# One more chunk of w_out's remainders on VectorE, two ScalarE steps moved to later units, and the order main, rest in the last sums and stores

## The chip, the cores and the metric

The kernel runs on one core of one Trainium2 chip. The metric is the device time of one execution in microseconds (us); 1128.37 us is the median of three runs of the kernel before. Durations below come from one profiled execution of it.

## The reference, cut to what matters

```python
w = softmax(weight_gen, axis=-1)                # (4, 4096, 8 heads, 7 taps)
x_unf[b, s, k] = x_pad[b, s + k]                # 7 causal taps over the sequence, zeros ahead of it
x = einsum('bshk,bskhg->bshg', w, x_unf)        # dynamic convolution, 24 channels a head
x = x.reshape(16384, 192)
h = x @ w_in                                    # (192, 2048)
g = h * (1.0 / (1.0 + exp(-1.702 * h)))
out = g @ w_out                                 # (2048, 192)
```

All inputs and outputs are float32.

## The kernel before, in words

The 16384 tokens are cut into 18 pieces: four narrow ones (512 tokens) and fourteen wide ones (1024 tokens). The hidden dimension is worked off in units. A unit is a 128-row chunk of the hidden dimension for 1024 columns; a narrow piece has 8 units and holds two chunks side by side in each, a wide one has 16. Unit n counts over the whole program, 0 to 255; v counts within a piece.

Matmuls take float32r operands, so each float32 operand is split in a rounded part (hi) and a remainder (lo = value - hi), and a product is hi*hi + hi*lo + lo*hi. For w_in (w1 in the code) and w_out (w2) this split is made in the kernel, in the first units, while the products already run. w2 has 16 chunks, held as two groups q of eight; the narrow pieces' unit n uses chunk n of both groups. A chunk of w2 is 192 columns: 128 for the main accumulator, 64 for the rest accumulator. "One chunk" in an index range like `w2_of(first, last, ...)` always means that chunk in both groups.

TensorE, per unit: `first_product(n)` (L633, the matmuls of L663, 18 pairs into hid) and, two units later, `second_product(n - 2)` (L667, matmuls of L679, 20 into acc_main and acc_rest). Its order at the start is first products 0, 1, 2, second 0, first 3, second 1, first 4, second 2, first 5, second 3, first 6, second 4, first 7, second 5, 6, 7, first 8. `second_product(n)` waits for unit n's `gate_lo`, and in its first units for the remainders of w2 (L683 to L686).

ScalarE, per unit: gate (L318) and gate_hi (L321) from hid, in order; behind them in certain units come extra steps. Unit 0: it rounds w2's chunks 4 to 7. Units 2 and 4: it copies two quarters of w1's late remainders into w1_lo (L333). Unit NEG_AT = 2: it writes the negated rounded chunks SOON to 7 of w2 (L337). Unit ADDED_AT = 5: it waits for the two transfers below and rounds their result into w2's remainder columns (L343), main and rest. VectorE, per unit: gate_lo (L577), then shares of the convolution of the pieces to come, in the order of a written list (STEPS_AT, STREAM); in unit 2 also `w2_remainder(2, 4)` (L470).

GpSimd only issues transfers there. After the negation (w2_negated) it issues two accumulating transfers (L608), one for each q, that add the negated rounded chunks to the raw ones and so leave raw - rounded; a similar one for w1's late half is issued at 14.3 us (L605). SyncE issues, in order: w1_hi doubled across the halves (L211, L212), w1_lo doubled (L215, L216) once `w1_late_ready` is 2, the taps of all later pieces (L200) once w2_lo_ready and w2_late_ready are complete, because they overwrite the raw weights, and then the windows of x (L248) and the output stores.

The last piece's last three units (REST_FIRST = 13) sum rest crosswise, main straight, rest straight, main crosswise. The end is then: ScalarE copies acc_rest's upper half (L358), VectorE adds the lower one (L561), ScalarE copies both main halves (L362), and stores go out as rest 0, main 0, rest 1 on SyncE (L236 to L243) and main 1 on ScalarE's queue (L364). All other units use main straight, rest crosswise, main crosswise, rest straight.

Of the kernel before, what the change touches and what calls it, by code (L numbers as in the profile page):

```python
# [5 lines left out]
P = 128  # L6
# [3 lines left out]
ACT = mybir.ActivationFunctionType  # L10
AX_X = mybir.AxisListType.X

HALF = 64
LANES = 32
NARROW, WIDE = 8, 16
PIECES = 4 * (NARROW,) + 14 * (WIDE,)
N = WIDE * LANES
# [1 line left out]
LAG = 2  # L19
SLOTS = 4  # L20
EVICT_AT = 1
REST_FIRST = 13
NEG_AT, ADDED_AT = 2, 5
MAX_AT, EXP_AT = 2, 3

STEPS_AT = ((0, 3, 5, 2, 4, 2, 2, 2),
# [12 lines left out]
def ffn_of_dynamic_conv(nc: bass.Bass, x_runs: bass.AP, tap_runs: bass.AP, x_first: bass.AP, tap_first: bass.AP,  # L39
# [15 lines left out]
    CH, D = w2_rows.shape[1:]  # L55
# [11 lines left out]
    LAST = len(PIECES) - 1  # L67
    START = [sum(PIECES[:j]) for j in range(len(PIECES) + 1)]
# [5 lines left out]
    with ExitStack() as ctx:  # L74
# [76 lines left out]
        def wait(eng, s, value):  # L151
            if value > 0:
                eng.wait_ge(s, value)
# [18 lines left out]

            return (k + h) % SLICES

        SOON = CH // 4
        LATE = slice(FH // 2, FH)
        MAIN, MAIN_LO = slice(0, P), slice(2 * P, 3 * P)
        REST_COLS, REST_HI, REST_LO = slice(P, 2 * P), slice(P, D), slice(D, 2 * P)
# [3 lines left out]

        def turned(j):
            return prod[:, 1, 0:PIECES[j] * CB].rearrange("p (k n) -> p k n", k=SLICES)

        def last_cols(h):
            return slice(2 * LANES * START[LAST] + h * N, 2 * LANES * START[LAST] + (h + 1) * N)

        def own(j, part):

# [6 lines left out]
        @block.sync  # L197
        def _(sp):
            def load_taps(first, last, s):
                sp.dma_start(taps[:, tap_span(first, last)], tap_runs[:, tap_span(first, last)]).then_inc(s, 16)  # L200

            sp.dma_start(taps[:, tap_span(0, 0)], tap_first).then_inc(taps_loaded[0], 16)
            sp.dma_start(x_head, x_first).then_inc(x_loaded, 16)
            sp.dma_start(w1_raw, w1_rows).then_inc(w1_loaded, 16)
            sp.dma_start(w2_raw, w2_rows).then_inc(w2_loaded, 16)
            sp.dma_start(ident[:], identity).then_inc(ident_loaded, 16)
            load_taps(1, 3, taps_loaded[1])
            sp.dma_start(xwin[:, 0:NARROW + HALO, :], x_runs[:, START[1]:START[2] + HALO, :]).then_inc(x_added, 16)

            sp.wait_ge(w1_hi_ready, 1)  # L210
            sp.dma_start(w1_hi[LOWER, :, 1, :].bitcast(F32), w1_hi[UPPER, :, 0, :].bitcast(F32)).then_inc(w1_doubled, 16)  # L211
            sp.dma_start(w1_hi[UPPER, :, 1, :].bitcast(F32), w1_hi[LOWER, :, 0, :].bitcast(F32)).then_inc(w1_doubled, 16)  # L212
            sp.wait_ge(w1_lo_ready, 3)
            sp.wait_ge(w1_late_ready, 2)
            sp.dma_start(w1_lo[LOWER, :, 1, :].bitcast(F32), w1_lo[UPPER, :, 0, :].bitcast(F32)).then_inc(w1_doubled, 16)  # L215
            sp.dma_start(w1_lo[UPPER, :, 1, :].bitcast(F32), w1_lo[LOWER, :, 0, :].bitcast(F32)).then_inc(w1_doubled, 16)  # L216
            sp.wait_ge(w2_lo_ready, 4)
            sp.wait_ge(w2_late_ready, 2)
            load_taps(4, LAST, taps_loaded[2])

            def store(j):
                cols = slice(2 * LANES * START[j], 2 * LANES * START[j + 1])
                if is_narrow(j):
                    sp.wait_ge(main_summed, j + 1)
                    sp.wait_ge(main_out_dve, j + 1)
                    sp.dma_start(out[0:P, cols], outs_main[:, 0, :]).then_inc(main_stored, 16)
                    sp.wait_ge(rest_summed, 2 * (j + 1))
                    sp.dma_start(out[P:D, cols], outs_rest[:, 0, :]).then_inc(rest_stored, 16)
                else:
                    sp.wait_ge(main_out_act, j + 1)  # L230
                    sp.wait_ge(main_out_dve, j + 1)
                    sp.dma_start(out[0:P, cols], outs_main[:].rearrange("p h n -> p (h n)")).then_inc(main_stored, 16)
                    sp.wait_ge(rest_out, 2 * (j + 1))
                    sp.dma_start(out[P:D, cols], outs_rest[:].rearrange("p h n -> p (h n)")).then_inc(rest_stored, 16)

            def store_last():  # L236

                sp.wait_ge(rest_out, 2 * LAST + 1)
                sp.dma_start(out[P:D, last_cols(0)], outs_rest[:, 0, :]).then_inc(rest_stored, 16)
                sp.wait_ge(main_out_act, LAST + 1)  # L240
                sp.dma_start(out[0:P, last_cols(0)], outs_main[:, 0, :]).then_inc(main_stored, 16)
                sp.wait_ge(rest_out, 2 * LAST + 2)
                sp.dma_start(out[P:D, last_cols(1)], outs_rest[:, 1, :]).then_inc(rest_stored, 16)  # L243

            def load_window(j):

                sp.wait_ge(conv_ready, j - 1)
                sp.dma_start(xwin[:], x_runs[:, START[j]:START[j] + WIN, :]).then_inc(x_reloaded, 16)  # L248

            load_window(2)  # L250
            for j in range(LAST):
                if j + 2 <= LAST and j >= 2:
                    load_window(j + 2)
                store(j)
            store_last()
            sp.wait_ge(main_stored, 16 * (LAST + 2))
            sp.wait_ge(rest_stored, 16 * (LAST + 2))

        @block.scalar
        def _(act):  # L260
# [50 lines left out]
            for j in range(LAST + 1):  # L311
                for v in range(UNITS[j]):
# [36 lines left out]
                    if is_narrow(j) and is_narrow(j + 1):  # L349
                        if v == CROSS_HI_AT[j]:  # L350
                            cross_rounded(j + 1)
                        if v == CROSS_LO_AT[j]:
                            cross_remainders(j + 1)

            act.wait_ge(rest_added, UNIT0[LAST + 1])
            act.wait_ge(rest_stored, 16 * LAST)
            for h in range(2):
                nc.scalar.activation(outs_rest[:, h, :], acc_rest[HALF:P, h, :], ACT.Copy).then_inc(rest_crossed, 1)  # L358
            act.wait_ge(main_added, UNIT0[LAST + 1])
            act.wait_ge(main_stored, 16 * LAST)  # L360
            for h in range(2):
                nc.scalar.activation(outs_main[:, h, :], acc_main[:, h, :], ACT.Copy).then_inc(main_out_act, 1)  # L362
            act.wait_ge(main_out_act, LAST + 2)
            act.dma_start(out[0:P, last_cols(1)], outs_main[:, 1, :]).then_inc(main_stored, 16)  # L364

        SOFTMAX_STEPS = 4
        ORDER = [("mul", 0), ("mul", 1)]
# [58 lines left out]
        def _(dve):  # L426
# [38 lines left out]
                        split_piece(j)  # L465

            def w2_remainder(first, last):
                dve.wait_ge(w2_hi_ready, last // 2)
                for to, of in ((MAIN_LO, MAIN), (REST_LO, REST_HI)):
                    nc.vector.tensor_tensor(w2_of(first, last, to), w2_of(first, last, of, w2_raw),  # L470
                                            w2_of(first, last, of), ALU.subtract).then_inc(w2_lo_ready, 1)
# [99 lines left out]
            for j in range(LAST + 1):  # L571
                for v in range(UNITS[j]):
# [7 lines left out]
                        maxima_and_shift(1)  # L580
                        maxima_and_shift(2)
                    if n == 2:
                        w2_remainder(2, SOON)
                    if v == MAX_AT and 1 <= j <= LAST - 2:
                        maxima_and_shift(j + 2)
                    first = steps_done
                    steps_done = min(first + STEPS_AT[kind(j)][v], len(STREAM))
                    prepare(first, steps_done)
            evict_rest(LAST)

        @block.gpsimd
        def _(pool):
# [20 lines left out]
        def _(pe):  # L613
# [53 lines left out]
            def second_product(j, v):  # L667
# [12 lines left out]
                                                start=start, stop=stop)  # L680
                    return done

                if n in (0, 2):  # L683
                    pe.wait_ge(w2_lo_ready, n + 2)
                if n == SOON:
                    pe.wait_ge(w2_late_ready, 2)  # L686
# [2 lines left out]
                    wait(pe, main_out_act, j)  # L689
                    wait(pe, main_out_dve, j)  # L690

                def straight_main():
                    wait(pe, main_added, n)
                    halves(acc_main, gate_hi, MAIN, False, first, False)
                    halves(acc_main, gate_hi, MAIN_LO, False, False, False)
                    halves(acc_main, gate_lo, MAIN, False, False, False).then_inc(main_straight, 1)

                def crosswise_rest():
                    if first:
                        wait(pe, rest_out, 2 * j)  # L700
                    wait(pe, rest_added, n)
                    halves(acc_rest, gate_hi, REST_COLS, True, first, False)
                    halves(acc_rest, gate_lo, REST_COLS, True, False, False).then_inc(rest_crosswise, 1)

                def crosswise_main():
                    wait(pe, main_straight, n + 1)
                    halves(acc_main, gate_hi, MAIN, True, False, False)
                    halves(acc_main, gate_hi, MAIN_LO, True, False, False)
                    halves(acc_main, gate_lo, MAIN, True, False, last_unit).then_inc(main_added, 1)

                def straight_rest():
                    wait(pe, rest_crosswise, n + 1)
                    halves(acc_rest, gate_hi, REST_COLS, False, False, False)
                    halves(acc_rest, gate_lo, REST_COLS, False, False, last_unit).then_inc(rest_added, 1)

                if j == LAST and v >= REST_FIRST:
                    crosswise_rest()
                    straight_main()
                    straight_rest()
                    crosswise_main()  # L720
                else:
                    straight_main()
                    crosswise_rest()
                    crosswise_main()
                    straight_rest()

            turn_head()
            for j in range(LAST + 1):
# [61 lines left out]
```

## Time and profile before

| | us |
|---|---|
| median of 3 runs | 1128.37 (1128.15 to 1128.38) |
| profiled execution | 1128.01 |
| its span, first to last instruction | 1126.2 |
| TensorE busy | 1111.2 (99%) |
| VectorE busy | 801.1 (71%) |
| ScalarE busy | 622.1 (55%) |
| GpSimd busy | 10.5 (1%) |
| mean granted clock of TensorE | 0.999 of full speed |

Times in rows are from the span's start. L12 is line 12 of the kernel. PE is TensorE, PEld its weight loads, DVE VectorE, ACT ScalarE, POOL GpSimd, SPq SyncE's queue of issues. Note "[0.95 <-X]" in a row says that the engine was idle for 0.95 us before it and that X ended the wait.

### The profile page before, as it was taken

How to read it: one execution, taken by the hardware profiler on the slowest of the kernel's cores; microseconds unless marked ns; L12 is line 12 of the kernel's file. 1: busy time of each engine (PE TensorE's matmuls, PEld its weight loads, DVE VectorE, ACT ScalarE, POOL GpSimd, SP SyncE). 2: the span in 40 equal slices, each digit the busy share in tenths (PEclk: the TensorE clock that was granted, in tenths of full speed). 3: DMA queues.
4: the chain of work that ended last, by engine and by line, in shares of the span. 5: the costliest groups of instructions: out<-in, count | busy, mean ns of one | idle time of the engine just before them, and what ended most of it. 6: DMA issues, size and time to landing. Idle time of an engine off the chain costs nothing.

```text
span 1126.2 us, 21690 instructions
## 1 busy us (share of the span) xinstructions
PE 1111.2 (99%) x9748; PEld 914.0 (81%) x9748; DVE 801.1 (71%) x709; ACT 622.1 (55%) x659; POOL 10.5 (1%) x11
## 2 busy tenths in 40 slices
PE   6999999999999999999999999999999999999998
PEld 4788888888888888888888888888888888888886
DVE  7999988587685866859668496785858768586322
ACT  7767655565545655455464554645555555454543
POOL 2000000000000000000000000000000000000000
PEclk9999999999999999999999999999999999999999
DMA  8801010101001010010100101010010100100000
GB/s 274 238 16 54 15 54 1 39 29 40 29 1 40 29 40 29 1 52 17 40 29 13 56 1 40 29 40 29 1 40 29 40 29 1 40 29 1 29 1 29
DMA packets 9948, 43.46 MB, mean 39 GB/s; under 512 B 1088, under 2 KB 2368, under 8 KB 7552
## 3 DMA queue, kind: packets, MB, share of 16 engines
q1 hardware_dynamic: 8256, 40.24, 10.8%
q0 software_dynamic: 1456, 1.57, 0.9%
q8 instruction: 77, 1.26, 0.5%
q10 hardware_dynamic: 144, 0.26, 0.1%
q14 instruction: 15, 0.12, 0.0%
HBM read 24.77 MB, written 12.58 MB: 33 GB/s over the span
## 4 chain that ended last, share of the span: by engine, by line
PE 97%; DVE 1%; ACT 1%; DMA 0%; issue 0%; SPq 0%; DVEq 0%
PE hid L663 46%; PE acc_main L679 31%; PE acc_rest L679 20%; DMA gate<-in_x_first 0%; DVE hid L498 0%; DVE prod L492 0%; ACT gate_hi L321 0%; DVE gate_lo L577 0%; ACT gate L318 0%; DVE prod L415 0%; ACT w L272 0%; ACT L318 0%; ACT L263 0%; ACT outs_main L362 0%; PE acc_main L630 0%
## 5 line engine op out<-in xcount | busy, mean ns | idle before, releaser
L318 ACT ACTIVATE gate<-hid 128x1024 f32<-128x1024 f32 x256 | 263.1, 1028 | 481.1 <-PE hid L663 479.4
L577 DVE TENSOR_TENSOR gate_lo<-gate,gate_hi 128x1024 fp32r<-128x1024 f32 x256 | 312.8, 1222 | 262.6 <-ACT gate_hi L321 262.6
L663 PE MATMUL hid<-xt,w_hi 64*128 64x512 f32 x3072 | 431.4, 386 | 0.0
L663 PEld LDWEIGHTS hid<-xt,w_hi 64*128 64x128 f32 x3072 | 287.5, 184 | 61.7 <-ACT gate_hi L321 0.8
L679 PE MATMUL acc_main<-gate_hi,w 64*128 64x512 f32 x2048 | 315.7, 386 | 0.5 <-DVE gate_lo L577 0.5
L321 ACT ACTIVATE gate_hi<-hid 128x1024 fp32r<-128x1024 f32 x256 | 261.2, 1020 | 0.0
L679 PEld LDWEIGHTS acc_main<-gate_hi,w 64*128 64x128 f32 x2048 | 191.5, 184 | 41.7 <-DVE gate_lo L577 1.1
L663 PE MATMUL hid<-xt,w_lo 64*128 64x512 f32 x1536 | 215.8, 386 | 0.0
L679 PE MATMUL acc_rest<-gate_hi,w 64*128 64x512 f32 x1024 | 199.4, 386 | 0.0
L679 PE MATMUL acc_main<-gate_lo,w 64*128 64x512 f32 x1024 | 199.4, 386 | 0.0
L679 PE MATMUL acc_rest<-gate_lo,w 64*128 64x512 f32 x1024 | 199.3, 386 | 0.0
L663 PEld LDWEIGHTS hid<-xt,w_lo 64*128 64x128 f32 x1536 | 143.9, 184 | 30.2
L422 DVE TENSOR_TENSOR conv<-conv,prod 128x1536 f32<-128x1536 f32 (+1 forms) x102 | 164.3, 1611 | 0.6
L415 DVE TENSOR_TENSOR prod<-xwin,tap_norm 128x1536 f32<-128x1536 f32 (+1 forms) x102 | 162.9, 1611 | 1.3 <-ACT xt L277 0.6
L679 PEld LDWEIGHTS acc_main<-gate_lo,w 64*128 64x128 f32 x1024 | 95.9, 184 | 20.2
L679 PEld LDWEIGHTS acc_rest<-gate_lo,w 64*128 64x128 f32 x1024 | 95.9, 184 | 20.2
L679 PEld LDWEIGHTS acc_rest<-gate_hi,w 64*128 64x128 f32 x1024 | 95.9, 184 | 20.2
L556 DVE COPY outs_main<-acc_main 128x512 f32<-128x512 f32 x13 | 9.0, 692 | 38.0 <-PE acc_main L679 38.0
L561 DVE TENSOR_TENSOR outs_rest<-acc_rest,outs_rest 64x512 f32<-64x512 f32 x36 | 23.0, 677 | 11.1 <-ACT outs_rest L309 7.5
L440 DVE STREAM_TRANSPOSE prod<-conv 128x1536 f32<-128x1536 f32 (+1 forms) x17 | 27.7, 1631 | 0.1
L448 DVE TENSOR_TENSOR xt<-prod,xt 128x1536 fp32r<-128x1536 f32 (+1 forms) x17 | 27.4, 1611 | 0.3 <-ACT xt L269 0.2
L415 DVE TENSOR_TENSOR conv<-xwin,tap_norm 128x1536 f32<-128x1536 f32 (+1 forms) x17 | 27.4, 1611 | 0.1
(59 smaller groups left out, 226.7 us busy)
## 6 DMA issues: line engine op xcount, KB each, us to landing
xwin<-in_x_runs SPq DMA_DIRECT2D x15, 1056.0 KB, 5.0
out<-outs_main SPq DMA_DIRECT2D x13, 512.0 KB, 2.6
out<-outs_rest SPq DMA_DIRECT2D x13, 256.0 KB, 2.9
taps<-in_tap_runs SPq DMA_DIRECT2D x1, 3136.0 KB, 14.4
taps<-in_w_rows SPq DMA_DIRECT2D x2, 1536.0 KB, 9.6
w_hi<-w_hi SPq DMA_DIRECT2D x2, 768.0 KB, 9.3
w_lo<-w_lo SPq DMA_DIRECT2D x2, 768.0 KB, 8.8
out<-outs_main SPq DMA_DIRECT2D x5, 256.0 KB, 2.1
```

Of the source, the lines that this page charges most:

```text
L318: nc.scalar.activation(gate[:, v % 2, :, :], hid[:, v % 2, :, :], ACT.Gelu_apprx_sigmoid).then_inc(gate_ready, 1)
L321: nc.scalar.activation(gate_hi[:, v % SLOTS, :, :], hid[:, v % 2, :, :], ACT.Gelu_apprx_sigmoid).then_inc(gate_hi_ready, 1)
L415: nc.vector.tensor_tensor(to.rearrange("p (g c) -> p g c", c=GRP), xwin[:, at:at + u, :].rearrange("p t (h c) -> p (t h) c", c=GRP), norm[ ...
L422: nc.vector.tensor_tensor(acc, acc, prod[:, k % 2, 0:u * CB], ALU.add).then_inc(conv_ready if last else conv_op, 1)
L440: nc.vector.transpose(turned(j).rearrange("p k (u i) -> p u k i", i=LANES), conv[:, 0:PIECES[j] * CB].rearrange("p (u k c) -> p u k c", k= ...
L448: nc.vector.tensor_tensor(own(j, 1), turned(j), own(j, 0), ALU.subtract).then_inc(xt_lo_ready, 1)
L556: nc.vector.tensor_copy(outs_main[:, 1, :], acc_main[:, 1, :]).then_inc(main_out_dve, 1)
L561: nc.vector.tensor_tensor(outs_rest[:, h, :], acc_rest[0:HALF, h, :], outs_rest[:, h, :], ALU.add).then_inc(rest_out, 1)
L577: nc.vector.tensor_tensor(gate_lo[:, v % SLOTS, :, :], gate[:, v % 2, :, :], gate_hi[:, v % SLOTS, :, :], ALU.subtract).then_inc(gate_lo_r ...
L663: last = nc.tensor.matmul(hid[:, v % 2, h, :], w[rows, k if j else slice_of(h, k), q, f], xt[rows, j % 2, part, k, :], start=(i == 0), sto ...
L679: done = nc.tensor.matmul(acc[:, h, :], w2[rows, chunk[h], cols], g[rows, s, h, :], start=start, stop=stop)
```

## The change

`SOON` goes from 4 to 5 chunks: VectorE subtracts chunk 4's remainders itself, in its unit 4 (n == 4), and the way over ScalarE and GpSimd's transfers now covers chunks 5 to 7 in place of 4 to 7. `NEG_AT` goes from 2 to 4, `ADDED_AT` from 5 to 6 (units count from 0). TensorE waits for chunk 4 at `w2_lo_ready` 6 in second product 4 and for the transferred remainders in second product 5 in place of 4. The rest-first order of the last units goes; the end of the last piece uses the common functions `lift` and `evict`, with ScalarE copying main 0, VectorE main 1, then the rest halves, and all four stores on SyncE in the order main 0, main 1, rest 0, rest 1.

```diff
-REST_FIRST = 13
-NEG_AT, ADDED_AT = 2, 5
+NEG_AT, ADDED_AT = 4,6
-        SOON = CH // 4
+        SOON = 5
-            sp.wait_ge(w2_lo_ready, 4)
+            sp.wait_ge(w2_lo_ready, 6)
             sp.wait_ge(w2_late_ready, 2)
             load_taps(4, LAST, taps_loaded[2])
...
-                sp.wait_ge(rest_out, 2 * LAST + 1)
-                sp.dma_start(out[P:D, last_cols(0)], outs_rest[:, 0, :]).then_inc(rest_stored, 16)
-                sp.wait_ge(main_out_act, LAST + 1)
-                sp.dma_start(out[0:P, last_cols(0)], outs_main[:, 0, :]).then_inc(main_stored, 16)
-                sp.wait_ge(rest_out, 2 * LAST + 2)
-                sp.dma_start(out[P:D, last_cols(1)], outs_rest[:, 1, :]).then_inc(rest_stored, 16)
+                for h in range(2):
+                    cols = slice(2 * LANES * START[LAST] + h * N, 2 * LANES * START[LAST] + (h + 1) * N)
+                    sp.wait_ge(main_out_dve if h else main_out_act, LAST + 1)
+                    sp.dma_start(out[0:P, cols], outs_main[:, h, :]).then_inc(main_stored, 16)
+                for h in range(2):
+                    cols = slice(2 * LANES * START[LAST] + h * N, 2 * LANES * START[LAST] + (h + 1) * N)
+                    sp.wait_ge(rest_out, 2 * LAST + 1 + h)
+                    sp.dma_start(out[P:D, cols], outs_rest[:, h, :]).then_inc(rest_stored, 16)
...
-            act.wait_ge(rest_added, UNIT0[LAST + 1])
-            act.wait_ge(rest_stored, 16 * LAST)
-            for h in range(2):
-                nc.scalar.activation(outs_rest[:, h, :], acc_rest[HALF:P, h, :], ACT.Copy).then_inc(rest_crossed, 1)
-            act.wait_ge(main_added, UNIT0[LAST + 1])
-            act.wait_ge(main_stored, 16 * LAST)
-            for h in range(2):
-                nc.scalar.activation(outs_main[:, h, :], acc_main[:, h, :], ACT.Copy).then_inc(main_out_act, 1)
-            act.wait_ge(main_out_act, LAST + 2)
-            act.dma_start(out[0:P, last_cols(1)], outs_main[:, 1, :]).then_inc(main_stored, 16)
+            lift(LAST)
...
                     if n == 2:
-                        w2_remainder(2, SOON)
+                        w2_remainder(2, 4)
+                    if n == 4:
+                        w2_remainder(4, SOON)
...
-            evict_rest(LAST)
+            evict(LAST)
...
-                if n in (0, 2):
+                if n in (0, 2, 4):
                     pe.wait_ge(w2_lo_ready, n + 2)
                 if n == SOON:
                     pe.wait_ge(w2_late_ready, 2)
...
-                if j == LAST and v >= REST_FIRST:
-                    crosswise_rest()
-                    straight_main()
-                    straight_rest()
-                    crosswise_main()
```

`lift(j)` waits for main_added, copies main half 0, waits for rest_added and copies the two rest halves. `evict(j)` is `evict_main(j)` (waits for main_added, copies main half 1 for a wide piece) and then `evict_rest(j)` (adds the lower rest half to each copied one).

## Rows read from the trace of the kernel before

**Rows 1.** The page's part 4: the chain that ended last, by engine.
```profile
PE 97%; DVE 1%; ACT 1%; DMA 0%; issue 0%; SPq 0%; DVEq 0%
```

**Rows 2.** Timeline of TensorE, units 2 to 7: start us, us, engine, line, operation, tiles, count.
```profile
30.72 0.84 PE L663 MATMUL hid<-xt,w_hi 64*128 64x512 f32 x6
...
36.39 0.73 PE L679 MATMUL acc_main<-gate_hi,w 64*128 64x512 f32 x4 [0.52 <-DVE gate_lo L577]
...
40.95 0.73 PE L679 MATMUL acc_main<-gate_hi,w 64*128 64x512 f32 x4
...
45.41 0.62 PE L679 MATMUL acc_main<-gate_hi,w 64*128 64x512 f32 x4
...
49.97 0.62 PE L679 MATMUL acc_main<-gate_hi,w 64*128 64x512 f32 x4
```

**Rows 3.** Timeline of ScalarE, units 2 to 5.
```profile
29.61 1.49 ACT L337 ACTIVATE w<-w 128x1536 fp32r<-128x1536 f32 x1
...
32.80 1.04 ACT L318 ACTIVATE gate<-hid 128x1024 f32<-128x1024 f32 x1
...
34.60 0.88 ACT L333 ACTIVATE w_lo<-taps 128x768 fp32r<-128x768 f32 x1
...
39.32 1.58 ACT L343 ACTIVATE w<-taps 128x1024 fp32r<-128x1024 f32 x2 [0.95 <-DMA taps<-w]
```

**Rows 4.** Timeline of GpSimd: the issues of its accumulating transfers.
```profile
14.27 1.43 POOL L605 DMA_DIRECT2D taps<-w_lo  x1 [1.85 <-ACT w_lo L291]
31.41 2.59 POOL L608 DMA_DIRECT2D taps<-w  x2 [15.72 <-ACT w L337]
```

**Rows 5.** Timeline of SyncE: doubling of w1_hi and of w1_lo, a window of x.
```profile
12.47 0.73 SPq L211 DMA_DIRECT2D w_hi<-w_hi  x1
...
35.58 0.60 SPq L215 DMA_DIRECT2D w_lo<-w_lo  x1
...
104.64 0.34 SPq L248 DMA_DIRECT2D xwin<-in_x_runs  x1
```

**Rows 6.** Busy time by stretch: us, PE, PEld, DVE, ACT, POOL, PEclk, DMA share, GB/s.
```profile
105.60:106.00 0.40, 0.40 (x6) 0.32 (x6) 0.40 (x2) 0.00 (x0) 0.00 (x0) 1.00 1.85 275
```

**Rows 7.** DMA queues, 16.5 to 22 us: packets, MB, share of 16 engines.
```profile
q1 hardware_dynamic: 304, 1.18, 101.8%
```

**Rows 8.** DMA queues, 35 to 38 us.
```profile
q0 software_dynamic: 630, 0.47, 120.4%
```

**Rows 9.** DMA queues, 39.5 to 44 us.
```profile
q1 hardware_dynamic: 258, 0.99, 98.0%
```

**Rows 10.** DMA queues, 46 to 58.3 us: the later taps and a window of x.
```profile
q1 hardware_dynamic: 489, 4.35, 87.0%
```

**Rows 11.** Timeline of VectorE, units 2, 7 and 9.
```profile
30.17 1.02 DVE L470 TENSOR_TENSOR w<-taps,w 128x512 fp32r<-128x512 f32 x2
...
48.62 1.18 DVE L577 TENSOR_TENSOR gate_lo<-gate,gate_hi 128x1024 fp32r<-128x1024 f32 x1
...
59.63 0.95 DVE L415 TENSOR_TENSOR conv<-xwin,tap_norm 128x768 f32<-128x768 f32 x1
```

**Rows 12.** Timeline of all engines, the end.
```profile
1120.23 1.08 ACT L358 ACTIVATE outs_rest<-acc_rest 64x512 f32<-64x512 f32 x2 [4.18 <-PE acc_rest L679]
...
1120.48 0.39 PE L679 MATMUL acc_main<-gate_lo,w 64*128 64x512 f32 x2
1120.85 1.28 DVE L561 TENSOR_TENSOR outs_rest<-acc_rest,outs_rest 64x512 f32<-64x512 f32 x2 [3.55 <-ACT outs_rest L358]
...
1122.70 0.47 SPq L243 DMA_DIRECT2D out<-outs_rest  x1
```

**Rows 13.** The one line's instructions: the last store (L243).
```profile
DMA to landing us min/median/max: 3.1/3.1/3.1
```

**Rows 14.** The page's part 6: rest stores of one half.
```profile
out<-outs_rest SPq DMA_DIRECT2D x6, 128.0 KB, 2.3
```

**Rows 15.** Busy time by stretch, behind TensorE's last matmul.
```profile
1123.20:1125.00 1.80, 0.00 (x0) 0.00 (x0) 0.00 (x0) 0.00 (x0) 0.00 (x0) 0.50 0.94 331
```

More of the change, by code:

```diff
@@ L184, in turned @@
             return prod[:, 1, 0:PIECES[j] * CB].rearrange("p (k n) -> p k n", k=SLICES)
-        def last_cols(h):
-            return slice(2 * LANES * START[LAST] + h * N, 2 * LANES * START[LAST] + (h + 1) * N)
         def own(j, part):
@@ L467, in w2_remainder @@
             def w2_remainder(first, last):
-                dve.wait_ge(w2_hi_ready, last // 2)
+                dve.wait_ge(w2_hi_ready, (last + 1) // 2)
                 for to, of in ((MAIN_LO, MAIN), (REST_LO, REST_HI)):
@@ L690, in second_product @@
                     wait(pe, main_out_dve, j)
[L692 to L714, printed above, removed]
@@ L716, in second_product @@
-                if j == LAST and v >= REST_FIRST:
-                    crosswise_rest()
-                    straight_main()
-                    straight_rest()
-                    crosswise_main()
[L721 to L725, printed above, removed]
+                wait(pe, main_added, n)
+                halves(acc_main, gate_hi, MAIN, False, first, False)
+                halves(acc_main, gate_hi, MAIN_LO, False, False, False)
@@ new lines, in second_product @@
+                halves(acc_main, gate_lo, MAIN, False, False, False).then_inc(main_straight, 1)
+                if first:
+                    wait(pe, rest_out, 2 * j)
+                wait(pe, rest_added, n)
+                halves(acc_rest, gate_hi, REST_COLS, True, first, False)
+                halves(acc_rest, gate_lo, REST_COLS, True, False, False).then_inc(rest_crosswise, 1)
+                wait(pe, main_straight, n + 1)
+                halves(acc_main, gate_hi, MAIN, True, False, False)
@@ L727, in _ @@
+                halves(acc_main, gate_hi, MAIN_LO, True, False, False)
+                halves(acc_main, gate_lo, MAIN, True, False, last_unit).then_inc(main_added, 1)
+                wait(pe, rest_crosswise, n + 1)
+                halves(acc_rest, gate_hi, REST_COLS, False, False, False)
+                halves(acc_rest, gate_lo, REST_COLS, False, False, last_unit).then_inc(rest_added, 1)
             turn_head()
```

## The prediction

> **What bounds the kernel now.** I read the chain of waits first: TensorE holds 97% of it [rows 1], so an edit counts only if it moves TensorE's first products, its last ones, or what comes behind the last. Then I read the timelines of the first 60 us engine by engine, because w_out's remainders are made there, and the timeline of the last 8 us. In the start TensorE stands twice: 0.52 us at second product 3, for VectorE's gate_lo, and shortly at second product 4, which starts at 40.95, right behind ScalarE's rounding of the transferred remainders (39.32 + 1.58 = 40.90) [rows 2, 3]. From 45.41 on it runs without a gap that matters. So whatever delays it there stays to the end, and the question is at what time the remainders of chunks 5 to 7 are there.
>
> **The negation moved from unit 2 to unit 4.** In unit 2 it took 1.49 us [rows 3] and gate 3 came right behind it. Without it gate 3 and gate 4 come earlier. Gate 4 started at 32.80, while first product 4 ended at 30.72 + 0.84 = 31.56 [rows 2, 3], so it gains 1.2 us, and the copy of w1's late remainders behind it starts at 33.4 in place of 34.60 and ends at about 34.3. TensorE gets nothing of that: gate_lo 3 is queued on VectorE behind convolution steps, and its 0.52 us stay. But two things follow. SyncE issues the doubling of w1_lo when that copy ends, at 34.4 in place of 35.58 [rows 5]. And the negation now stands behind the copy on ScalarE: 1152 columns a partition in place of 1536, so 1.49 x 1152/1536 = 1.1 to 1.2 us, ended at about 35.3. GpSimd issued 0.3 us behind its end (29.61 + 1.49 = 31.10, 31.41) [rows 3, 4], so now at 35.65, which is 1.25 us after SyncE's issue. Before, GpSimd was first by 4.2 us.
>
> **What the order of issue costs.** The trace shows twice what happens when two queues meet. GpSimd's transfer for w1 was issued at 14.27, 1.8 us behind the first doubling of w1_hi at 12.47 [rows 4, 5]; from 16.5 to 22 us only q1, SyncE's queue, moved anything [rows 7]. Nearly 6 us it stood behind what was issued before it. The other way round, the doubling of w1_lo was issued at 35.58, and until 38 us only q0, GpSimd's queue, moved anything [rows 8], though a transfer of SyncE with free engines moves bytes 1.0 to 1.4 us after its issue (104.64 to 105.6 or a little later) [rows 5, 6]. Both times the earlier issue was served out first. So I take first come, first served:
> - The doubling of w1_lo starts at 34.4 + 1.1 = 35.5. It is 2 x 768 KB = 1.57 MB, at 0.99 MB in 4.5 us (0.22 MB/us) [rows 9] 7.2 us: to 42.7.
> - GpSimd's two transfers then have 3/4 of 786 KB = 0.59 MB, at 0.47 MB in 3 us [rows 8] 3.8 us: to 46.5. ScalarE saw the transfers before at 39.32, some 0.5 us after their last packets: 47.0.
> - ScalarE waits in unit 6, in front of its rounding: before 1.58 us for 1024 and 512 columns [rows 3], now 768 and 384. By the 0.88 us of the 128x768 copy [rows 3] and half of that, 1.25 us: 48.25.
> - Second product 5 starts 0.05 us later, at 48.3. Before it started at 45.41 [rows 2]: 2.9 us. A start after a wait costs a little more (0.73 us for the first four matmuls in place of 0.62 [rows 2]): 3.0 us. Its early end at second product 4, up to 0.25 us, is swallowed by this wait.
>
> Bounds of this term: if the doubling starts 0.3 us later, or either rate is 5% lower, it is 3.6; with everything the other way 2.5. I keep 3.0.
>
> Queued behind the waiting rounding on ScalarE are gate 7 and gate_hi 7: 48.25 + 2 us, then VectorE's gate_lo 7, to 51.5. Second product 7 starts two second products (4.56 us by 45.41 and 49.97 [rows 2]) behind 48.4, at 53.0, so they are in time, and so is the rounding of piece 1 (0.9 us) behind them: first product 8 comes only at 55.3.
>
> **One chunk more on VectorE.** Two subtractions of 256 and 128 columns in unit 4. In unit 2, 512 and 256 columns took 1.02 us [rows 11], so half as many about 0.55. VectorE has no idle time there; gate_lo 7, which ran 48.62 to 49.80, would end at 50.35. Second product 7 started at 49.97 [rows 2]. Without the long wait that would cost TensorE 0.4 us and a restart of 0.13; with it, second product 7 starts at 53.0 and it costs nothing. It lets second product 4 run without ScalarE, worth nothing as said.
>
> **The transfers behind.** SyncE sends the later taps (3136 KB) only after the rounding, at 48.3, and the window of piece 2 (1056 KB) behind them: 4.29 MB from 49.4 on, at 4.35 MB in 12.3 us [rows 10] 12.1 us, landed by 62.1. VectorE wants the window at 59.63 + 3.0 = 62.6 [rows 11]. It holds by 0.5 us; where it doesn't, the late step pushes gate_lo 10, which ScalarE and TensorE's second product 10 need some 4 us later, so it costs nothing.
>
> **The end.** TensorE's last matmul still ends at 1120.48 + 0.39 = 1120.87 [rows 12] in before's time, but main is ready 4 matmuls earlier, at 1120.42 (20 matmuls of a second product last 2.27 us). ScalarE copies main 0 to 1121.0 while VectorE copies main 1 to 1121.15. The rest is ready at 1120.87; ScalarE's two copies (1.08 us [rows 12]) end at 1122.15, and VectorE's two adds, which start 0.62 us behind ScalarE's first copy and take 1.28 us [rows 12], run 1121.7 to 1122.97. So the last store is issued at 1123.0 in place of 1122.70 [rows 12]. But before, it landed 3.1 us after its issue [rows 13], with main 1 on ScalarE's queue just ahead of it; now only rest 0, issued 0.6 us earlier, is ahead, and such stores land in 2.3 us as a rule [rows 14], say 2.4. 1123.0 + 2.4 = 1125.4 against 1125.8: -0.35 us; bounds -0.6 and +0.3 (landing 3.1 as before).
>
> **The clock.** Behind the last matmul (1120.87) the granted clock was down to half, 1.2 GHz, by 1123.2, after 2.3 us without work [rows 12, 15]. TensorE's wait at second product 5 lasts from first product 7's end at 45.2 to 48.3, so a fall is about as likely as not. The trace has no matmul at half clock. From below it costs nothing; if the clock took as long to come back as to fall, 2.3 us of matmuls would do the work of 1.15 us, a loss of 1.1. I take 0.5.
>
> **Sum.** 3.0 - 0.35 + 0.5 = +3.15 us on the profiled execution of 1128.01 (span 1126.2 and 1.8 around it), 1131.15; its median is 0.36 above it, so 1131.5.
>
> **Rivals.**
> - Shared engines: the queues take turns, each at half rate. GpSimd's packets come at 35.65 + 1.8 = 37.45 and take 7.6 us in place of 3.8: 45.05, seen at 45.55, rounded by 46.8, second product 5 at 46.85, +1.55 with the restart; no fall of the clock, the end -0.35: 1129.6. Against it is that neither meeting in the trace showed turns [rows 7, 8]; for it, that both began with one queue well ahead.
> - Not slower: GpSimd's queue is served when it comes, wherever SyncE's stands. Seen at 37.45 + 3.8 + 0.5 = 41.75; the rounding comes behind gate and gate_hi 6, 2 us that begin when first product 6 ends, just before 40.95 [rows 2], so it is done at 44.2, before first product 7 ends at 45.2. Then VectorE's chunk decides, +0.55 at second product 7, and the end gives 0.35: 1128.6. It decides when the remainders are seen by 43.9. Against it: 16.5 to 22 us [rows 7].
> - The wait is as forecast and the clock stays down for longer than it took to fall, or the doubling is slower beside the rest: 1133.5.
>
> The Trainium skill's DMA: Bandwidth & Descriptors (Queues, rings and completion order) states the first of these: each DMA engine takes the queue rows in turn, a packet of many descriptors at a time. By that rule the time would be 1129.6, by the rows 1131.5. The trace doesn't agree where it can be seen: 304 packets of one queue in 5.5 us and none of the other, which had been issued.
>
> **How the numbers follow.** First come first served 0.75, shared 0.13, not slower 0.07, longer than forecast 0.05. The forecast's own range is 2.5 - 0.6 + 0 to 3.6 + 0.3 + 1.1, so 1130.3 to 1133.4, its ends together unlikely. The range given takes in the shared case and leaves out the not slower one, and above it ends a little inside: 1129.4 to 1133.0. What can be told from no change is 0.2%, 2.3 us, so slower begins at 1130.6: the forecast case but for its lowest end (0.67), and the last rival (0.05): 0.72; within 0.2% the rest of the forecast case (0.08) and the two other rivals but for a tenth of them, 0.26; faster that tenth, 0.02.
>
> **What would show it.** The rounding L343 with an idle time of 4 us before it, ended by GpSimd's transfer, and starting near 47.0; w1_lo's issue near 34.4 and GpSimd's near 35.65; q1 alone from 36 to 42 us, q0 alone for 3.8 us after it; TensorE idle for about 3 us before second product 5, and from there every row later by about 3 us; VectorE's L470 a third time, 0.55 us in unit 4, without a wait of TensorE on it; PEclk below 1.00 for a few us near 48 or not at all; the last store issued about 0.3 us later against the last matmul and landed in 2.4. I am wrong if L343 starts before 45, or if GpSimd's issue comes before SyncE's.

## The result: 5.8 us slower, by the mechanism that was forecast and nearly twice its size

| | median us | runs | ratio to before, 95% interval |
|---|---|---|---|
| before | 1128.34 | 6 | |
| changed | 1134.16 (1133.60 to 1135.01) | 6 | 1.0052 (1.0039 to 1.0065) |

The forecast was 1131.5, its range 1129.4 to 1133.0. The profiled execution of the changed kernel took 1134.49 us, its span 1132.7, against 1128.01 and 1126.2.

Line numbers moved: L653 is the first products' matmul (before L663), L669 the second's (L679), L341 the rounding of the remainders (L343), L335 the negation (L337), L598 GpSimd's issue (L608), L565 gate_lo (L577), L458 VectorE's remainders (L470), L211 and L212 the doubling of w1_lo (L215, L216).

First ScalarE's timeline of the changed kernel in units 4 to 7, to be read against [rows 3]:
```profile
33.31 0.85 ACT L331 ACTIVATE w_lo<-taps 128x768 fp32r<-128x768 f32 x1
34.05 1.17 ACT L335 ACTIVATE w<-w 128x1152 fp32r<-128x1152 f32 x1
...
48.24 1.26 ACT L341 ACTIVATE w<-taps 128x768 fp32r<-128x768 f32 x2 [5.40 <-DMA taps<-w]
```
The copy is earlier, the negation behind it, and the rounding stood 5.40 us for GpSimd's transfers. SyncE's and GpSimd's issues, against [rows 4, 5]: SyncE is now first, by 1.3 us.
```profile
34.25 0.59 SPq L211 DMA_DIRECT2D w_lo<-w_lo  x1
```
```profile
35.52 2.57 POOL L598 DMA_DIRECT2D taps<-w  x2 [19.95 <-ACT w L335]
```
The DMA queues of the changed kernel from 36 to 42 us, and from 43.5 to 46 us (packets, MB, share of 16 engines), against [rows 7, 8]:
```profile
q1 hardware_dynamic: 334, 1.30, 98.8%
```
```profile
q0 software_dynamic: 576, 0.43, 122.8%
...
q1 hardware_dynamic: 2, 0.00, 0.0%
```
Until 42 us SyncE's queue had all engines though GpSimd had issued at 35.52; from 43.5 on GpSimd's had them. Between 42.4 and 43.4 us both moved bytes, as one went out and the other came in. From 42.5 to 43 us:
```profile
q0 software_dynamic: 41, 0.03, 51.1%
q1 hardware_dynamic: 16, 0.03, 35.1%
```
TensorE's timeline at second products 5 to 7, against [rows 2]:
```profile
44.33 0.84 PE L653 MATMUL hid<-xt,w_hi 64*128 64x512 f32 x6
49.55 1.22 PE L669 MATMUL acc_main<-gate_hi,w 64*128 64x512 f32 x4 [4.38 <-ACT w L341]
50.57 0.63 PE L669 MATMUL acc_main<-gate_lo,w 64*128 64x512 f32 x2
...
55.50 0.62 PE L669 MATMUL acc_main<-gate_hi,w 64*128 64x512 f32 x4
...
58.95 0.87 PE L653 MATMUL hid<-xt,w_hi 64*128 64x512 f32 x6
```
Two losses stand there. Second product 5 starts at 49.55 in place of 45.41, 4.14 us late. And a pair took 0.63 us from its first start to its last end instead of 0.39. The busy time by stretch shows why; the third number from the right is the granted clock:
```profile
47.00:47.80 0.80, 0.00 (x0) 0.00 (x0) 0.80 (x2) 0.00 (x0) 0.00 (x0) 1.00 0.09 12
48.00:49.00 1.00, 0.00 (x0) 0.00 (x0) 0.97 (x2) 0.76 (x2) 0.00 (x0) 0.50 0.00 0
50.00:54.00 4.00, 4.00 (x22) 3.01 (x22) 2.58 (x3) 2.90 (x4) 0.00 (x0) 0.50 0.88 307
55.00:58.00 3.00, 3.00 (x28) 2.47 (x26) 0.40 (x2) 0.17 (x1) 0.00 (x0) 1.00 1.11 477
```
The clock fell to 1.2 GHz near 47.9, 2.8 us behind first product 7's last matmul (45.17), and came back near 54.8: 22 matmuls in 4 us, then 28 in 3. Second products 5 to 7 took 58.95 - 49.55 = 9.40 us; before, between the same two points, 52.23 - 45.41 = 6.82. So 2.58 us are the clock's and the restart's. All six executions have a mean clock of 0.996 to 0.998, against 0.999 and 1.000 in the kernel before, so it fell in each of them.

The end, against [rows 12]:
```profile
1127.43 0.60 ACT L303 ACTIVATE outs_main<-acc_main 128x512 f32<-128x512 f32 x1 [4.50 <-PE acc_main L669]
1127.43 0.69 DVE L544 COPY outs_main<-acc_main 128x512 f32<-128x512 f32 x1 [3.24 <-PE acc_main L669]
1127.45 0.39 PE L669 MATMUL acc_rest<-gate_lo,w 64*128 64x512 f32 x2
...
1128.68 1.28 DVE L549 TENSOR_TENSOR outs_rest<-acc_rest,outs_rest 64x512 f32<-64x512 f32 x2 [0.56 <-ACT outs_rest L307]
1129.39 1.11 SPq L241 DMA_DIRECT2D out<-outs_rest  x2
```
TensorE's last matmul ends at 1127.84, the span at 1132.7: 4.86 us, against 1126.2 - 1120.87 = 5.33.

The sum: 4.14 + 2.58 at the wait, 0.25 spread over TensorE's other work (1127.84 - 1120.87 = 6.97 in all), -0.47 at the end: 6.50, and the spans differ by 6.5.

### The profile page after: what moved, and what is told of

Read it like the earlier page. It is cut to its first block, busy times and chain, and to the rows that moved or that the text cites. A ratio compares the mean times of both kernels' runs of the same rounds, so it can differ in the third digit from the quotient of the medians.

```text
span 1132.7 us, 21693 instructions
## 1 busy us (share of the span) xinstructions
PE 1114.0 (98%) x9748; PEld 917.6 (81%) x9748; DVE 802.6 (71%) x712; ACT 621.0 (55%) x658; POOL 10.5 (1%) x11
## 4 chain that ended last, share of the span: by engine, by line
PE 97%; DMA 1%; DVE 1%; ACT 0%; issue 0%; POOL 0%; ACTq 0%; DVEq 0%; SPq 0%
PE hid L653 46%; PE acc_main L669 31%; PE acc_rest L669 20%; DMA taps<-w 1%; DMA gate<-in_x_first 0%; DVE hid L486 0%; DVE prod L480 0%; PE acc_main L620 0%; ACT w L335 0%; ACT gate L316 0%; DVE hid L480 0%; ACT gate_hi L319 0%; POOL taps L598 0%; DVE outs_main L508 0%; ACTq L73 0%
## 5 line engine op out<-in xcount | busy, mean ns | idle before, releaser
L565 DVE TENSOR_TENSOR gate_lo<-gate,gate_hi 128x1024 fp32r<-128x1024 f32 x256 | 312.9, 1222 | 265.2 <-ACT gate_hi L319 265.2
L653 PE MATMUL hid<-xt,w_hi 64*128 64x512 f32 x3072 | 431.6, 386 | 0.0
L653 PEld LDWEIGHTS hid<-xt,w_hi 64*128 64x128 f32 x3072 | 288.2, 184 | 61.0 <-ACT gate_hi L319 0.8
L669 PE MATMUL acc_main<-gate_hi,w 64*128 64x512 f32 x2048 | 317.3, 388 | 4.9 <-ACT w L341 4.4
L669 PEld LDWEIGHTS acc_main<-gate_hi,w 64*128 64x128 f32 x2048 | 192.6, 185 | 46.1 <-ACT w L341 4.8
L653 PE MATMUL hid<-xt,w_lo 64*128 64x512 f32 x1536 | 215.9, 386 | 0.0
L669 PE MATMUL acc_rest<-gate_lo,w 64*128 64x512 f32 x1024 | 200.1, 387 | 0.0
L669 PE MATMUL acc_rest<-gate_hi,w 64*128 64x512 f32 x1024 | 200.1, 387 | 0.0
L669 PE MATMUL acc_main<-gate_lo,w 64*128 64x512 f32 x1024 | 200.0, 387 | 0.0
L653 PEld LDWEIGHTS hid<-xt,w_lo 64*128 64x128 f32 x1536 | 144.2, 184 | 29.9
L669 PEld LDWEIGHTS acc_main<-gate_lo,w 64*128 64x128 f32 x1024 | 96.5, 185 | 20.2
L669 PEld LDWEIGHTS acc_rest<-gate_hi,w 64*128 64x128 f32 x1024 | 96.4, 185 | 20.2
L669 PEld LDWEIGHTS acc_rest<-gate_lo,w 64*128 64x128 f32 x1024 | 96.4, 185 | 20.2
```

What stands on the lines that cost most here:

```text
L565: nc.vector.tensor_tensor(gate_lo[:, v % SLOTS, :, :], gate[:, v % 2, :, :], gate_hi[:, v % SLOTS, :, :], ALU.subtract).then_inc(gate_lo_r ...
L653: last = nc.tensor.matmul(hid[:, v % 2, h, :], w[rows, k if j else slice_of(h, k), q, f], xt[rows, j % 2, part, k, :], start=(i == 0), sto ...
L669: done = nc.tensor.matmul(acc[:, h, :], w2[rows, chunk[h], cols], g[rows, s, h, :], start=start, stop=stop)
```

## The experiments

Theory: a transfer that is issued behind another one is served behind it, so the late negation costs the whole service of w1_lo's doubling, and the wait that it makes lets the clock fall. Rivals: the later negation or GpSimd's slow path costs by itself; VectorE's chunk costs; the queues share; the slow matmuls are due to the load of the taps.

**Only the new end.** The changed kernel with SOON 4, NEG_AT 2, ADDED_AT 5 and the waits that go with them:
```diff
-NEG_AT, ADDED_AT = 4,6
+NEG_AT, ADDED_AT = 2, 5
-        SOON = 5
+        SOON = CH // 4
```

> The start of the kernel before with the end of the changed one (SOON 4, negation in unit 2, rounding in unit 5; last sums and stores in the order main, rest). In the traces the time from TensorE's last matmul to the end of the span is 1126.2 - 1120.87 = 5.33 us before and 1132.7 - 1127.84 = 4.86 us after. Theory (the end gains, the start loses): 0.47 us less than before, 1127.9 us. Rival (the difference at the end is chance, of one execution each): 1128.3 us, and a tail of 5.3 us again. If the new end were what made the change slow, 1134.

Measured: 1127.95 us (11 runs) beside 1128.30 of before, ratio 0.9998 (0.9989 to 1.0006). The profiled one ends its last matmul at 1120.73 + 0.40 = 1121.13 and its span at 1126.0: 4.87 us, as in the changed kernel. The tail is shorter by 0.46 us in the trace, and the medians agree with that; the interval alone doesn't tell it from nothing.

**Only the new start.** The kernel before with SOON 5, NEG_AT 4, ADDED_AT 6 and their waits.

> The kernel before with only the start changed (SOON 5, negation in unit 4, rounding in unit 6); last sums and stores stay in the order rest, main. Theory (the two parts of the change add up, since TensorE has no slack between them): the changed kernel plus what the new end gave alone, 1134.16 + 0.35 = 1134.5 us, and from TensorE's last matmul to the end of the span 5.3 us as before. Rival (the end's gain was chance or depends on the start): 1134.2 us or less.

Measured: 1134.33 us (5 runs), ratio 1.0052 (1.0037 to 1.0066). The last matmul ended at 1127.82, the span at 1133.2: 5.4 us, as before. The whole loss is in the start. That the medians of this kernel and the changed one differ by only 0.2 says nothing against 0.4, since each spreads by 1.4 to 2 us.

**The negation back in unit 2.** The rest of the change stays.
```diff
-NEG_AT, ADDED_AT = 4,6
+NEG_AT, ADDED_AT = 2, 6
```

> The changed kernel with the negation back in unit 2 (chunk 4 still on VectorE, rounding still in unit 6, new end). Theory (GpSimd's transfers stood behind SyncE's doubling of w1_lo because they were issued after it): GpSimd issues near 31.1 us, before SyncE's 35.4, its transfers are seen by 38, L341 has no DMA wait, TensorE stands at second product 5 for nothing and the clock does not fall. What is left is VectorE's 0.6 us for the chunk, late at second product 7 by 0.5, and the end's -0.5: 1128.3 us. Rival (VectorE's chunk or the later unit of the rounding costs most of the 5.8 us): 1131 or more.

Measured: 1128.37 us (11 runs), ratio 1.0000 (0.9991 to 1.0009). GpSimd issued at 31.38, SyncE at 35.55. ScalarE's timeline has no DMA wait at the rounding, and TensorE's only wait behind it is for VectorE:
```profile
43.16 1.26 ACT L341 ACTIVATE w<-taps 128x768 fp32r<-128x768 f32 x2
```
```profile
50.68 0.73 PE L669 MATMUL acc_main<-gate_hi,w 64*128 64x512 f32 x4 [0.39 <-DVE gate_lo L565]
```
All of the loss is gone, with the chunk still on VectorE and the rounding still in unit 6. What the chunk costs, with the rounding a unit later, is seen against the run with only the new end: 1128.37 - 1127.95 = 0.4 us.

**The negation late, the doubling later.** SyncE's wait and its two transfers of w1_lo (L211, L212) move behind the window of piece 2; nothing else changes.
```diff
-            sp.wait_ge(w1_lo_ready, 3)
-            sp.wait_ge(w1_late_ready, 2)
-            sp.dma_start(w1_lo[LOWER, :, 1, :].bitcast(F32), w1_lo[UPPER, :, 0, :].bitcast(F32)).then_inc(w1_doubled, 16)
-            sp.dma_start(w1_lo[UPPER, :, 1, :].bitcast(F32), w1_lo[LOWER, :, 0, :].bitcast(F32)).then_inc(w1_doubled, 16)
...
             load_window(2)
+            sp.wait_ge(w1_lo_ready, 3)
...
```

> The changed kernel with the negation left in unit 4, and only SyncE's doubling of w1_lo moved behind its taps and the window of piece 2. Theory (the place behind the doubling costs, not the late negation): GpSimd issues at 35.5 as before this edit, its transfers have the DMA engines to themselves, 1.8 us until the first packet, 3.8 us of service, 0.5 us to be seen: 41.6 us, hidden behind gate_hi 6. No wait at second product 5, clock stays at full, 1128.3 us as in the run with the negation in unit 2. Rival (the negation 4.1 us later brings the remainders that much later whatever else is in the queues, since GpSimd's path is slow): the remainders seen at 44 or later, some us of wait, 1130 to 1134.

Measured: 1128.50 us (11 runs), ratio 1.0001 (0.9992 to 1.0010). GpSimd issued at 36.07, as late as in the changed kernel; each of its two transfers landed 4.3 and 6.2 us after its issue, against 10.5 and 11.9. The DMA queues from 37 to 42 us, and the rounding without a wait:
```profile
q0 software_dynamic: 788, 0.58, 90.2%
...
taps<-w POOLq DMA_DIRECT2D x2, 288.0 KB, 5.2
```
```profile
43.28 1.25 ACT L341 ACTIVATE w<-taps 128x768 fp32r<-128x768 f32 x2
```
So a negation 4.7 us later costs nothing with nothing ahead of it in the engines. The rival of GpSimd's slow path falls. There was little to spare, though: the second transfer was issued at 36.9 and landed at 43.1, not at 41.6 as expected, and ScalarE came to the rounding at 43.28. 0.6 us of that is the later issue, and most of the rest is a last engine. Most of q0's bytes had been moved by 41.9, and from 42.0 to 42.3 us, and again from 42.3 to 42.6, the queue still shows
```profile
q0 software_dynamic: 5, 0.00, 8.8%
```

**Half of the doubling ahead.** Only the second of the two transfers moves behind the window.

> The changed kernel with the first doubling of w1_lo (768 KB) in its place and the second moved behind the window of piece 2. Theory (each transfer issued ahead is served out first, so the wait is linear in the bytes ahead): half of the 7.3 us of service ahead goes, the remainders are seen 3.6 us earlier, near 44.6 in place of 48.2, rounded by 45.9; second product 5 starts 0.7 us late, no fall of the clock, and second product 7 is held by VectorE's chunk at about the same time; 1128.6 to 1129.2 us. Rival (the queues take turns at their packets once both have work, and the second doubling behind the first costs nothing by itself): 1131 or more.

Measured: 1128.70 us (11 runs), ratio 1.0009 (1.0000 to 1.0017). The rounding started at 44.47, 3.8 us earlier than in the changed kernel, near the 44.6 expected:
```profile
44.47 1.26 ACT L341 ACTIVATE w<-taps 128x768 fp32r<-128x768 f32 x2 [1.00 <-DMA taps<-w]
```
Seven of the eleven took 1128.3 to 1128.9, where the theory has them, and four 1130.2 to 1131.1, near the rival's 1131. Three of the four have a mean clock of 0.999 or 1.000, so a fall of the clock does not explain these. No profile shows one of the four, so their cause stays open.

**Work inside the wait.** The changed kernel with matmuls into hid's slot 0, which has been read by then; FILL is 17, 12 and 6 in three kernels.
```diff
                 if n == SOON:
+                    pe.wait_ge(gate_hi_ready, UNITS[0] - 1)
+                    for i in range(FILL):
+                        for h in range(2):
+                            rows = slice(h * HALF, (h + 1) * HALF)
+                            nc.tensor.matmul(hid[:, 0, h, :], w1_hi[rows, i % SLICES, 0, 0:P], xt[rows, 0, 0, i % SLICES, :],
+                                             start=True, stop=True)
                     pe.wait_ge(w2_late_ready, 2)
```

> The changed kernel with 34 matmuls more (17 pairs, their results are overwritten) on TensorE in front of its wait at second product 5: 34 x 0.1135 = 3.9 us of work inside a wait of 4.38. The remainders come as late as in the changed kernel. Theory (2.4 of its 5.8 us are the clock at half from 48 to 54.6 us, because TensorE stood idle): the clock stays at full, second products 5 to 7 take 6.8 us in place of 9.4, 1131.8 us. Rival (these matmuls are slow because the taps and the window of x are loaded at 350 to 450 GB/s at that time, or because of the restart): they stay at 9.4 us, 1134.2 us.

> The changed kernel with 24 filler matmuls in front of the wait: 2.7 us of work, 1.7 us of idle time left. The clock fell 2.8 us behind the last matmul in the changed kernel's wait, and 2.1 and 2.3 us behind it at the two kernels' ends, so 1.7 us should be too short: 1131.9 us as with 34 matmuls. If the length of the idle time did not matter but only whether it is there, 1134.

> The changed kernel with 12 filler matmuls in front of the wait: 1.4 us of work, 3.0 us of idle time left. Longer than the 2.1 to 2.8 us after which the clock fell in three places, so it should fall in this wait too, but later against the wait's end: 1133.5 to 1134.5 us, and in some executions more than in others. If any work inside the wait kept the clock up, 1131.9.

Measured: 1131.91 us with 34 matmuls (5 runs, ratio 1.0033, 1.0020 to 1.0045), 1131.37 with 24 (7 runs), 1131.37 with 12 (5 runs, one of them 1133.44). TensorE's timeline and one stretch of the kernel with 34:
```profile
45.17 4.01 PE L681 MATMUL hid<-xt,w_hi 64*128 64x512 f32 x34
49.38 0.73 PE L670 MATMUL acc_main<-gate_hi,w 64*128 64x512 f32 x4 [0.20 <-ACT w L342]
...
56.41 0.84 PE L654 MATMUL hid<-xt,w_hi 64*128 64x512 f32 x6
```
```profile
50.00:54.00 4.00, 4.00 (x38) 3.25 (x36) 2.74 (x3) 2.74 (x4) 0.00 (x0) 1.00 0.95 332
```
The remainders come as late (the rounding starts at 48.07), the taps are loaded at much the same rate (332 GB/s beside 307), and second products 5 to 7 take 56.41 - 49.38 = 7.03 us, not 9.40; 38 matmuls in the 4 us that had 22. The slow matmuls were the clock, not the loads. It also shows the two losses apart: of 5.8 us, 2.25 are the clock by the medians (1134.16 - 1131.91), 2.37 by this stretch (9.40 - 7.03), and 2.8 by the medians with 24 and 12. The rest, 3.0 to 3.6 us, is the wait less the end's gain.

With 24 matmuls TensorE stood 1.65 us and the clock stayed. With 12 I expected it to fall, and in the profile it did not; there the transfers were seen early, so TensorE stood only for 1.96 us:
```profile
47.16 1.26 ACT L342 ACTIVATE w<-taps 128x768 fp32r<-128x768 f32 x2 [4.33 <-DMA taps<-w]
```
Only the run of 1133.44 has a lower mean clock (0.998 against 0.999 to 1.000) and is 2 us slower. The 1133.5 to 1134.5 expected was missed. The expectation took 2.1 to 2.8 us, from three places, for the time after which the clock falls; the other traces, in the last section, show up to 5.1 us.

**The chunk back on the long way.** The changed kernel with SOON 4, so that second product 4 waits; negation and rounding stay late.

> The changed kernel with SOON 4 again: chunk 4 goes over the negation in unit 4, GpSimd's transfers and the rounding in unit 6, so second product 4 waits for it in place of second product 5. Theory (the chunk on VectorE is what keeps the late negation from costing a unit more): the transfers are a third larger, seen at 49.5, rounded by 51.1, second product 4 starts 10.1 us later than before, the clock falls for 5 us of work or more (2.4 us), the end gives 0.5: 1140 us. Rival (the wait depends on the service only, and the place at which TensorE waits is of no matter): 1135.5 us.

Measured: 1139.76 us (4 runs), ratio 1.0102 (1.0088 to 1.0115). ScalarE's and TensorE's timelines:
```profile
49.40 1.57 ACT L341 ACTIVATE w<-taps 128x1024 fp32r<-128x1024 f32 x2 [6.24 <-DMA taps<-w]
```
```profile
51.03 1.22 PE L667 MATMUL acc_main<-gate_hi,w 64*128 64x512 f32 x4 [9.85 <-ACT w L341]
```
Second product 4 starts 10.1 us later (51.03 against 40.95), as expected, so the chunk on VectorE saves the late order 5.6 us. In a kernel whose transfers are on time it costs 0.4.

## Why the prediction was wrong in size

- **Order of issue, right.** SyncE's issue was put at 34.4 and came at 34.25; GpSimd's at 35.65, came at 35.52; q1 alone, then q0 alone. Two kernels that undo that order, one by the negation's place and one by the doubling's, bring the time back to 1128.4 and 1128.5.
- **The service behind it, mis-sized: 3.0 us forecast, 4.1 measured.** This is the first step that failed. The remainders were to be seen at 47.0 and were at 48.24. The step "3.8 us: to 46.5" divided GpSimd's bytes by the rate of all 16 engines; the wait ends with the last engine. The changed kernel's q0 from 47 to 48 us:
```profile
q0 software_dynamic: 15, 0.01, 7.5%
```
  A share of 7.5% is one engine (with all 16 at work from 43.5 to 46 us it was 122.8%, 7.7% for each): it worked a microsecond longer than the rest, which had ended by 46.5 or so. In the kernel with 12 fillers q0 had nothing from 47 us on, and its rounding started at 47.16. Over five profiles of this order (47.16, 48.07, 48.24, 48.49, 48.51) the forecast's 47.0 lies just below the earliest. The kernel with the doubling moved back has a late engine too, of 0.7 us, with nothing ahead of the transfers; so the doubling ahead is not what makes it. What does was not tried.
- **The clock, mis-sized: 0.5 us forecast with a bound of 1.1, 2.3 measured.** That it could fall was right. The step that failed is "if the clock took as long to come back as to fall": it fell 2.8 us after the last matmul and came back 5.2 us after work had begun again. Half of 5.2 is 2.6; the stretch shows 2.4. With this term and the one above at their measured sizes the sum is 1131.5 + 1.1 + 1.8 = 1134.4, and 1134.16 was measured.
- **VectorE's chunk, right:** 0.62 us in unit 4, hidden by the wait; 0.4 where the wait is gone. The forecast for the "not slower" rival, 1128.6, is what the two kernels without the wrong order took (1128.4, 1128.5).
- **The transfers behind, right in that nothing came of them:** taps and window were issued at 49.57 and 49.96.
- **The end, right:** -0.35 forecast, -0.47 in the traces.
- **The rival of shared queues**, which the Trainium skill's DMA: Bandwidth & Descriptors (Queues, rings and completion order) states as a rule, would have given 1129.6. The rows above disagree with the rival as it was priced, turns at half rate from 37.45 on: 334 packets of one queue in 6 us and none of the other, which had been issued. They don't refute the rule itself, and the prediction's "The trace doesn't agree" says too much. By that section of the Trainium skill an engine drains a whole packet of typically 9 to 17 descriptors, at most 64, before it switches, while the profile's packets are single rows of 4 KB: the two doublings together are 384 such rows, 24 for each of 16 engines. A turn that holds them all would look just like this. So what is shown is that two transfers of this size, issued 1.3 and 0.6 us ahead, were served out first. Whether the engines go by the order of issue, stay with a queue until it is empty, or take long turns, no run here tells apart.

Among all kernels here the one with the old start and the new end is the fastest (1127.95), by an amount that its interval doesn't tell from before.

## What to carry to other kernels

Moving a producer later can cost far more than the move: GpSimd's issue came 4.1 us later (35.52 against 31.41), and the remainders 8.9 us later (48.24 against 39.32). Look at which transfers it falls behind, and count their whole service, to the last engine, as ahead of it. Where TensorE's wait is longer than the 1.65 and 1.96 us that left the clock up here, add the clock as a term of its own, because the half rate goes on into the work behind the wait. If such a wait can't be avoided, matmuls whose results are thrown away, put inside it, gave back 2.3 to 2.8 us of 5.8 here.

## What had not been expected of the hardware

- How long TensorE stood before its granted clock fell differs widely. It fell 2.8 us after the last matmul in the changed kernel's wait (45.17 to 47.94) and 2.3 us after it in the wait of the kernel with only the new start. In the kernel with the chunk on the long way it took 5.1 us: the last matmul ended at 41.18, and the clock is the third number from the right in
```profile
46.10:46.20 0.10, 0.00 (x0) 0.00 (x0) 0.10 (x1) 0.00 (x0) 0.00 (x0) 1.00 1.18 161
46.30:46.40 0.10, 0.00 (x0) 0.00 (x0) 0.10 (x1) 0.00 (x0) 0.00 (x0) 0.50 1.45 192
```
  At the ends of the kernels it fell 2.0 us (only the new start) to 4.8 us (chunk on the long way) after the last matmul, and with 12 fillers not at all in 4.9 us. The waits of 1.65 and 1.96 us that left it up are shorter than any of these, the second by next to nothing.
- It came back 5.2 us after work had begun again in the changed kernel, 4.8 us after in the one with only the new start (49.82 to 54.6), and 5.4 us after in the one with the chunk on the long way (51.03 to near 56.5, mean clock 0.77 from 56 to 57 us).
- A lead of 1.3 us in issue, 0.6 us for the second of two transfers, was enough to put one queue's 1.57 MB ahead of the other's: GpSimd's landed 10.5 and 11.9 us after their issue behind SyncE's, 4.3 and 6.2 us after it with nothing ahead.
